# Three places in a buffer of the first MLP's activation where there were four, four buffers in turn where there were three, and another order around the last projection

## The reference

```python
# attention with a forget gate: B, H, S, D = 4, 8, 768, 48
state = f[:, :, t, :, None] * state + einsum('bhd,bhe->bhde', k_t, v_t)
y[:, :, t] = einsum('bhd,bhde->bhe', q_t, state)
# x: 3072 tokens x 384
h = x @ w_in                      # 384 -> 2048
x = (h * tanh(log1p(exp(h)))) @ w_out          # mish, 2048 -> 384
x = (sigmoid(x @ w_gate) * (x @ w_val)) @ w_out2   # 384 -> 1536 -> 384
```

## Time and profile before

| | us |
|---|---|
| three runs | 1015.27, 1015.95, 1018.53 |
| median | 1015.95 |
| profiled execution | 1016.86 |
| its span, first to last instruction | 1014.7 |
| PE busy in it | 988.7 |
| DVE busy | 534.3 |
| ACT busy | 521.5 |
| POOL busy | 134.5 |

### The profile page before, as it was taken

The page is one execution under the profiler, slowest core; times in us unless marked ns, Lnnn a source line. Parts: engine busy times, 40 slices in busy tenths (PEclk is TensorE's granted clock), DMA queues, the critical chain, the costliest instruction groups (busy, mean ns, idle before and its releaser), DMA issues.

```text
span 1014.7 us, 14110 instructions
## 1 busy us (share of the span) xinstructions
PE 988.7 (97%) x4885; PEld 817.6 (81%) x4885; DVE 534.3 (53%) x760; ACT 521.5 (51%) x883; POOL 134.5 (13%) x150
## 2 busy tenths in 40 slices
PE   5999999999999999999999999999999999999997
PEld 4988898888878888778887888888888888888886
DVE  7999996776676776687777422222222222222221
ACT  3676677888787887777777321112221112221112
POOL 2333235000000000034555400000000000000000
PEclk9999999999999999999999999999999999999999
DMA  5666641000000000011111100000100000000001
GB/s 194 202 209 197 208 135 48 17 1 1 1 1 0 0 0 0 0 31 47 47 47 47 39 1 1 1 1 0 63 0 0 0 0 31 31 1 1 1 1 63
DMA packets 36492, 42.27 MB, mean 42 GB/s; under 512 B 2912, under 2 KB 24928, under 8 KB 36448
## 3 DMA queue, kind: packets, MB, share of 16 engines
q1 hardware_dynamic: 36448, 41.69, 13.3%
HBM read 36.96 MB, written 4.72 MB: 41 GB/s over the span
## 4 chain that ended last, share of the span: by engine, by line
PE 87%; DVE 6%; issue 4%; ACT 2%; DMA 1%; DVEq 0%; ACTq 0%
PE banks L877 28%; PE banks L879 27%; PE banks L878 27%; PE banks L903 2%; DVE suffix L683 2%; DVE prefix L700 2%; PE banks L918 2%; PE banks L923 1%; PE banks L908 0%; DVE state L731 0%; PE banks L933 0%; DVE probs L717 0%; ACT qt L505 0%; DMA out_dram<-rows_out 0%; DVE glo L673 0%
## 5 line engine op out<-in xcount | busy, mean ns | idle before, releaser
L877 PE MATMUL banks<-xhi,whi 128*128 (+1 forms) x720 | 284.5, 395 | 0.0
L879 PE MATMUL banks<-xhi,wlo 128*128 (+1 forms) x720 | 283.0, 393 | 0.0
L878 PE MATMUL banks<-xlo,whi 128*128 (+1 forms) x720 | 280.5, 390 | 0.0
L877 PE MATMUL banks<-ghi,whi 128*128 128x512 f32 x504 | 199.8, 396 | 5.3 <-DVE glo L673 5.0
L843 DVE TENSOR_TENSOR prod<-prod,banks 128x512 f32<-128x512 f32 x72 | 49.5, 687 | 290.2 <-PE banks L879 290.2
L879 PE MATMUL banks<-ghi,wlo 128*128 128x512 f32 x504 | 197.7, 392 | 0.0
L878 PE MATMUL banks<-glo,whi 128*128 128x512 f32 x504 | 196.4, 390 | 0.0
L879 PEld LDWEIGHTS banks<-xhi,wlo 128*128 128x128 f32 x720 | 135.1, 188 | 32.2
L878 PEld LDWEIGHTS banks<-xlo,whi 128*128 128x128 f32 x720 | 135.3, 188 | 30.8
L877 PEld LDWEIGHTS banks<-xhi,whi 128*128 128x128 f32 x720 | 135.1, 188 | 28.6
L585 ACT ACTIVATE prod<-banks 128x512 f32<-128x512 f32 x72 | 43.1, 598 | 187.6 <-PE banks L879 187.6
(11 more groups left out here) (72 smaller groups left out, 953.2 us busy)
## 6 DMA issues: line engine op xcount, KB each, us to landing
xb<-f_dram SPq DMA_DIRECT2D x24, 256.0 KB, 3.1
kb<-k_dram SPq DMA_DIRECT2D x24, 256.0 KB, 3.2
qb<-q_dram SPq DMA_DIRECT2D x24, 256.0 KB, 3.6
raw<-w_out_dram SPq DMA_DIRECT2D x28, 192.0 KB, 2.4
vb<-v_dram SPq DMA_DIRECT2D x24, 192.0 KB, 2.4
out_dram<-rows_out SPq DMA_DIRECT2D x15, 256.0 KB, 2.2
raw<-w_in_dram SPq DMA_DIRECT2D x16, 192.0 KB, 2.7
raw<-w_gate_dram SPq DMA_DIRECT2D x12, 192.0 KB, 2.4
```

What stands on the lines that cost most here:

```text
L877: pe.matmul(ps, hi, xh, start=first, stop=False)
L878: pe.matmul(ps, hi, xl, start=False, stop=False)
L879: return pe.matmul(ps, lo, xh, start=False, stop=last)
```

## The change

A buffer of `sets` gets three places instead of four, and there are four buffers instead of three: NSET = 4. Both take 12 x 512 columns. `shifted` writes to place 0, where the tanh was, and therefore waits for `silu_done` too. `prod` keeps three buffers, under the new name NPROD. With NSET = 4, POS1 is 32, so no place of a pass is empty. At the end of the last pass the gate of the second MLP's first unit is issued before the projection of unit 30 and the value behind it, each with its own condition on `silu_done`.

```diff
-NSET = 3
+NSET = 4
+NPROD = 3
...
-        sets = sb("sets", [P, NSET, 4, TILE], F32, at)
+        sets = sb("sets", [P, NSET, 3, TILE], F32, at)
...
-        prod = sb("prod", [P, NSET, TILE], F32, at)
+        prod = sb("prod", [P, NPROD, TILE], F32, at)
...
                 act.wait_ge(m.square_done, p * N1 + i + 1)
-                act.activation(st[:, 3], st[:, 2], ACT.Square, bias=shift_bias).then_inc(m.shifted_done, 1)
+                act.wait_ge(m.silu_done, p * N1 + i + 1)
+                act.activation(st[:, 0], st[:, 2], ACT.Square, bias=shift_bias).then_inc(m.shifted_done, 1)
...
-                dve.scalar_tensor_tensor(st[:, 3], st[:, 3], Z_SHIFT, st[:, 2], ALU.add, ALU.mult).then_inc(m.cubic_done, 1)
+                dve.scalar_tensor_tensor(st[:, 0], st[:, 0], Z_SHIFT, st[:, 2], ALU.add, ALU.mult).then_inc(m.cubic_done, 1)
...
-                op = dve.scalar_tensor_tensor(st[:, 1], st[:, 3], MISH_K, st[:, 1], ALU.subtract, ALU.mult, reverse0=True)
+                op = dve.scalar_tensor_tensor(st[:, 1], st[:, 0], MISH_K, st[:, 1], ALU.subtract, ALU.mult, reverse0=True)
...
-            def gate_val(p, i):
+            def gate_val(p, i, products=range(2)):
                 j, t = i // TP, i % TP
                 cols = bass.ds(p * PASS + t * TILE, TILE)
-                for m in range(2):
+                for m in products:
...
                 if isinstance(p, int) and (p, i) == (NPASS, 0):
 
-                    pe.wait_ge(silu_done, NPASS * N1)
-                    gate_val(0, 0)
+                    pe.wait_ge(silu_done, NPASS * N1 - 1)
+                    gate_val(0, 0, (0,))
                 for lag, do in ((0, hidden), (LOOK, project)):
...
                     if at := lag_b(p, i, lag):
                         do(*at)
+                if isinstance(p, int) and (p, i) == (NPASS, 0):
+                    pe.wait_ge(silu_done, NPASS * N1)
+                    gate_val(0, 0, (1,))
```

More of the change, by code:

```diff
@@ L163, in attention_mlp_mlp @@
         wlo2 = sb("wlo2", [P, EXTRA, DM], F32R, at)
-        assert at[0] <= shared + NSET * 4 * TILE * 4, at
+        assert at[0] <= shared + NSET * 3 * TILE * 4, at
         at = [top_of_glo]
@@ L583, in sigmoid @@
                 act.wait_ge(gate_done, p * N2 + i + 1)
-                wait(act, p_ready, p * N2 + i + 1 - NSET)
-                act.activation(prod[:, i % NSET], h_ps[0][:, :], ACT.Sigmoid).then_inc(sig_done, 1)
+                wait(act, p_ready, p * N2 + i + 1 - NPROD)
+                act.activation(prod[:, i % NPROD], h_ps[0][:, :], ACT.Sigmoid).then_inc(sig_done, 1)
             def product_high(p, i):
@@ L589, in product_high @@
                 wait(act, acc2_done, p * N2 + i - 1)
-                act.activation(ghi[:, i % 2], prod[:, i % NSET], ACT.Copy).then_inc(phi_done, 1)
+                act.activation(ghi[:, i % 2], prod[:, i % NPROD], ACT.Copy).then_inc(phi_done, 1)
             def mish(p, i):
@@ L842, in product @@
                 dve.wait_ge(sig_done, p * N2 + i + 1)
-                dve.tensor_tensor(prod[:, i % NSET], prod[:, i % NSET], h_ps[1][:, :], ALU.mult).then_inc(p_done, 1)
+                dve.tensor_tensor(prod[:, i % NPROD], prod[:, i % NPROD], h_ps[1][:, :], ALU.mult).then_inc(p_done, 1)
                 dve.wait_ge(phi_done, p * N2 + i + 1)
-                dve.tensor_tensor(glo[:, i % 2], prod[:, i % NSET], ghi[:, i % 2].bitcast(F32),
+                dve.tensor_tensor(glo[:, i % 2], prod[:, i % NPROD], ghi[:, i % 2].bitcast(F32),
                                   ALU.subtract).then_inc(p_ready, 1)
```

## The result

The changed kernel takes 1019.13 us (median of 20 runs, 1015.78 to 1021.23) where the kernel before takes 1015.81 (20 runs, 1014.55 to 1018.72): a ratio of 1.0028, 95% interval 1.0020 to 1.0037. By the medians that is 3.3 us more (0.33%), by the ratio 2.8 us (0.28%): the 0.3% up to which I had called it "the same" lies between the two.

The account below looks back on a forecast made before the run. PE, busy 97%, was taken as the bound, so only its waits could move. Plus 1.72 us at two inner pass ends minus 0.89 at the last gave plus 0.83: 1016.8 us on the median 1015.95, range 1014.8 to 1018.9.

Parts of the forecast that it names:

- What bounds the kernel: PE is busy 97% of the 1014.7 us span; the change can move only PE's waits, at most 6.75 us.
- the pitch: Mid-pass, PE starts a hidden group of nine matmuls every 4.146 us; the change should leave this as it is.
- the old waits: PE waits before projections: 0.79 and 1.53 us at each inner pass end (2.93 us in all), 0.89 at the last.
- Four buffers in turn: Fourth buffer of the hidden units' steps: its wait condition is met long before either way, so it gains nothing.
- the 0.79: PE's wait before unit 30's projection at each inner pass end, 0.79 us; said to go with the empty place.
- The wait for the sums: Inner pass ends: projection of u0 3.24 us late behind accumulator emptying, u1 then 0.44; 3.79 us per pass end.
- The extra wait of the shifted square: ACT's shifted square must wait for the product reading the tanh it overwrites; taken as 0, bounds 0 to 0.12 us.
- cover of 1.2 us: Time by which the shifted square, read at unit 31, starts after the product that it must wait for.
- my chain: Step-by-step reckoning of ACT's and DVE's queues at the first inner pass end, giving the projections of u0 and u1.
- Gate and value, minus 0.89: Last pass end: gate and value around unit 30's projection remove its wait, 0.89 us, and nothing comes for it.
- The sum: Plus 1.72 us at both inner pass ends, minus 0.89 at the last: plus 0.83 us.
- The clock rival: The longer wait at both inner pass ends makes TensorE's clock fall: 3.5 us for two falls, 1020.3 us; chance 8%.

Follow-up runs that it names:

- e2: The changed kernel with gate and value together again, behind the projection of unit 30: 1019.82 us, ratio 1.0041 to the kernel before.
- e3: The changed kernel with seven matmuls that nothing reads ahead of the projection of u0 at the inner pass ends: ratio 1.0018 to the kernel before.
- e10: The changed kernel with the same seven unread matmuls, run again beside the changed kernel on one chip: 1017.19 us, ratio 1.0018 to the kernel before.
- e5: The changed kernel with the empty place kept (33 places in a pass), buffers and extra wait as in the change: ratio 1.0008 to the kernel before.
- e1: The kernel before with only gate and value of the last pass end moved around the projection of unit 30: 1014.33 us against 1014.95, ratio 0.9995.
- e6: The changed kernel with two unread matmuls ahead of the projection of u0 at the inner pass ends: ratio 1.0019 to the kernel before.

## Why the prediction was right, and where it was wrong

- *What bounds the kernel, the pitch, the size of the old waits*: right. The pitch is 4.146 us before and after.
- *Four buffers in turn are worth nothing, the 0.79 before unit 30's projection goes*: right; the six groups up to 292.32 run through.
- *The wait for the sums behind two units' steps*: right. Forecast 3.24 us late and then 0.44 more, measured 3.21 and, where the clock stays up (e2, e3, e10), 3.97 per pass end in all against 3.79.
- *The extra wait of the shifted square, taken as 0 under a cover of 1.2 us*: mis-sized. The cover is that of the middle of a pass. At u2 the silu stands behind the subtractions, and there the wait is 0.17 us (e5: plus 0.17 per pass end). It is the missing 0.18 of 3.97 - 3.79. In e2 the projection of u1 comes 22.55 us behind the hidden group of unit 31, in my chain 22.34. I had read the cover from unit 31 and not looked where the silu comes latest.
- *Gate and value, minus 0.89*: right, 0.93 (e1).
- *The sum*: without the clock it is 2 x 1.04 - 0.93 = 1.15 us and some 0.1 in the first units; I had said 0.83. The two filled executions, e3 and e10, show this sum in the MLPs: 845.71 - 844.49 = 1.22 us.
- *The clock rival, 8%*: this is the step that failed. It happened in both profiled executions of the changed kernel, and 25 of the 32 runs are at a mean clock of 0.995 or less. Its price came out about right, 3.5 us said for two falls and 3.1 measured (changed kernel against e3), but the row that I took it from shows no fall: the first chunk of the attention is as slow (the row below this list), so TensorE was slow from its first matmul on, not because of the 2.46 us. That two falls cost nearly what I said is luck: one cost 0.9 us, the other 2.2. What was wrong was the chance, and the argument for it: I compared my wait of 3.08 us with one single fall, 2.85 to 3.05 us behind the last matmul, and took the one sample as a threshold that the wait would just miss. The sample lay below the wait, so it spoke for the fall. With an even chance for it the forecast would have stood between the two cases and the range reached 1020.3, the time that I had worked out for it.
- *Direction and size*: slower, as forecast, and "the same" by the bound of 0.3%, but barely: the ratio is 1.0028, and its interval reaches beyond 1.003. Most of the difference is what the forecast left out: of 4.28 us more in the MLPs of the profiled execution the clock makes 3.1. That the time came out at the edge of the range is owed to the room that the range had for one fall, and to the runs in which the clock fell less; it doesn't bear out the sum of 0.83.

The first chunk of the attention, in the trace of the kernel before:

```profile
9.92 3.75 PE L903 MATMUL banks<-qt,kb 128*128 128x256 f32 x8 [9.92 <-ACT qt L505]
```

What stays open: why the clock falls at one pass end and not at the next with the same idle stretch (e6), and before the burst or behind its start; and the 0.24 us of e5 outside of the inner pass ends, and the share of the fourth buffer in it, since e5 has the four buffers and their three places at once.

## What to carry to other kernels

When a bubble is taken out of a hand-written order, list every operation that was placed relative to it, here the emptying of the accumulators, and ask which of them now stands behind one more unit's steps: the gain of 6 us was only there once these subtractions moved along. Read the cover of a new wait at the place where its operand comes latest, not in the middle of the loop. And price a longer idle stretch of TensorE twice, by its own length and by what the clock takes behind it.

## What the runs showed of the hardware

- At the pass ends the granted clock went to 1.2 GHz in or right behind idle stretches of TensorE of 2.59 and 3.04 us, in part of the cases only, and never behind 1.45 to 1.6 us. In the changed kernel it stayed low for 3.4 us of work in one case (297.98 to 301.4) and for 6.1 us in the other (435.2 to 441.3). The Trainium skill, "TensorE: Matmul & The Clock Gate", section "HAM oscillation — how this bites in real kernels", describes this fall and the cold start behind it; the traces agree with both, but the gaps that it speaks of are longer than the 2.59 and 3.04 us here, and on that the traces decide.
- Idle time is not the whole of it. Early in the attention PE waits 2.46 us once, up to 15.9 to 17.0 us in the twelve traces. In eight of the twelve profiled executions the clock had come up by then, and in seven of these it fell again within 1.4 us behind that wait. In e3 it fell at 59.7 us, for 3.4 us, with no idle stretch over 0.63 us in the 25 us before.
- A fall does not cost what its slow matmuls cost. At the first pass end of the changed kernel eight matmuls stood 0.2 us further apart, 1.6 us, but the pass end grew by 4.88 - 3.97 = 0.91 only: the later wait, 0.43 us of idle time and the slow start behind it (e2), was gone. The projection of u1 began later, when the subtractions of unit 31's sums were through. At the second it was 6.13 - 3.97 = 2.16.
- The view of the granted clock says 1.00 from 9 to 22 us in the trace of the kernel before, where eight matmuls take 3.75 us that take 1.99 later: at the start of this trace the column doesn't show what the durations do.
